# A fused attention and expert kernel: the second dense step in seven-product form, the sums of x shared by VectorE and GpSimd

## The reference

```python
N, D, E, F = (1152, 512, 4, 1024)
p = domain_probs / (domain_probs.sum(-1, keepdims=True) + 1e-09)
out = np.zeros((N, D), dtype=np.float32)
for e in range(E):
    h = np.maximum(x @ w1[e], 0.0)
    out += p[:, e:e + 1] * (h @ w2[e])
```

## Time and profile before

| What | Value |
|---|---|
| Median of 3 runs | 610.3 us (609.96 to 613.1) |
| The profiled execution's own time | 610.63 us |
| Its span in the profile | 608.9 us |
| TensorE busy | 593.7 us, 98% of the span |
| VectorE, ScalarE, GpSimd busy | 346.9, 214.8, 305.4 us |
| Mean granted TensorE clock | 0.999 of full |

### The profile page before, as it was taken

The page is one execution under the profiler, slowest core; times in us unless marked ns, Lnnn a source line. Parts: engine busy times, 40 slices in busy tenths (PEclk is TensorE's granted clock), DMA queues, the critical chain, the costliest instruction groups (busy, mean ns, idle before and its releaser), DMA issues.

```text
span 608.9 us, 10251 instructions
## 1 busy us (share of the span) xinstructions
PE 593.7 (98%) x3607; PEld 524.0 (86%) x3608; DVE 346.9 (57%) x714; ACT 214.8 (35%) x542; POOL 305.4 (50%) x287
## 2 busy tenths in 40 slices
PE   4999999999999999999999999999999999999996
PEld 4898878888888889989889889899899899899894
DVE  4878775248892123785464564554554554654553
ACT  2867732258983231223123123122132132131130
POOL 6546601451110019359996945945756747646005
PEclk9999999999999999999999999999999999999999
DMA  9926556628951002002222112112112011010004
GB/s 213 249 36 238 198 176 236 212 86 302 357 220 35 18 17 71 1 0 70 70 69 71 36 34 70 36 36 69 34 35 69 26 43 60 15 63 0 0 0 155
DMA packets 27252, 56.70 MB, mean 93 GB/s; under 512 B 7000, under 2 KB 9688, under 8 KB 27224
## 3 DMA queue, kind: packets, MB, share of 16 engines
q1 hardware_dynamic: 18792, 31.93, 16.6%
q0 software_dynamic: 6848, 21.52, 10.8%
q10 hardware_dynamic: 1584, 2.88, 1.6%
HBM read 48.97 MB, written 7.36 MB: 93 GB/s over the span
## 4 chain that ended last, share of the span: by engine, by line
PE 91%; POOL 3%; DVE 2%; DMA 2%; issue 1%; ACT 0%; SPq 0%; DVEq 0%; POOLq 0%
PE bank L1618 30%; PE bank L1589 30%; PE bank L1513 10%; PE bank L1499 10%; PE bank L1396 2%; PE bank L1488 2%; POOL out L627 1%; PE bank L1433 1%; PE bank L1359 1%; PE bank L1407 1%; DMA kT<-in_kT 1%; PE bank L1476 1%; PE bank L1482 1%; PE bank L1391 1%; PE bank L1354 1%
## 5 line engine op out<-in xcount | busy, mean ns | idle before, releaser
L1263 DVE SCALAR_TENSOR_TENSOR acc<-bank,meta_s,acc 128x512 f32<-128x512 f32 x135 | 100.8, 748 | 62.2 <-PE bank L1618 62.1
L1618 PE MATMUL bank<-u_hi,h_hi 128*128 128x512 f32 x288 | 112.3, 390 | 0.0
L1618 PE MATMUL bank<-u_lo,h_hi 128*128 128x512 f32 x288 | 112.1, 389 | 0.0
L1618 PE MATMUL bank<-u_hi,h_lo 128*128 128x512 f32 x288 | 112.0, 389 | 0.0
L1310 DVE SCALAR_TENSOR_TENSOR h_lo<-bank,h_hi 128x288 fp32r<-128x288 f32 x112 | 50.9, 454 | 44.7 <-ACT h_hi L811 23.0
L1589 PE MATMUL bank<-x2T_hi,u_hi 128*128 128x288 f32 x232 | 68.4, 295 | 0.0
L1589 PE MATMUL bank<-x2T_lo,u_hi 128*128 128x288 f32 x232 | 68.4, 295 | 0.0
L1589 PE MATMUL bank<-x2T_hi,u_lo 128*128 128x288 f32 x232 | 68.3, 295 | 0.0
L799 ACT COPY part_p<-bank 128x288 f32<-128x288 f32 x28 | 11.2, 400 | 157.9 <-PE bank L1589 157.9
L1589 PE MATMUL bank<-t_hi,u_hi 128*128 128x288 f32 x224 | 66.2, 295 | 0.0
L1589 PE MATMUL bank<-t_lo,u_hi 128*128 128x288 f32 x224 | 66.0, 295 | 0.0
(11 more groups left out here) (235 smaller groups left out, 1222.7 us busy)
## 6 DMA issues: line engine op xcount, KB each, us to landing
w_raw<-in_moe_w SPq DMA_DIRECT2D x20, 1024.0 KB, 7.6
u_raw<-in_moe_w POOLq DMA_DIRECT2D x16, 512.0 KB, 3.8
u_raw<-in_moe_w POOLq DMA_DIRECT2D x16, 256.0 KB, 3.2
u_raw<-in_moe_w POOLq DMA_DIRECT2D x32, 128.0 KB, 2.9
x_tile<-x_by_expert ACTq DMA_DIRECT2D x11, 256.0 KB, 2.7
x_by_expert<-zero_row SPq DMA_DIRECT2D x10, 256.0 KB, 3.1
qT<-in_qT SPq DMA_DIRECT2D x4, 576.0 KB, 9.1
kT<-in_kT SPq DMA_DIRECT2D x8, 288.0 KB, 10.5
```

The source lines that it names most:

```text
L1263: w.scalar_tensor_tensor(out=acc[:, t, :], in0=bank[Z_BANK[i]][:], scalar=meta_s[:, t, bass.ds(e + 1, 1)], in1=acc[:, t, :], op0=ALU.mult, ...
L1618: last = t_.matmul(bank[Z_BANK[i]][:], lhs[:, c, ts], rhs[page][:, c, :], start=c == 0 and k == 0, stop=c == 1 and k == 2)
```

## The change

`PLAIN` becomes 1, so step 1 is a seven-product step too. Its differences of x must be there one step earlier:

- VectorE makes the eight sums of `x_sum[0]` itself, two behind each of four `cut_plain` of step 0, then the four `make_t` of `s = 0`; GpSimd makes only those of `x_sum[1]`, between `split_u1(1)` and `split_u2(1)`.
- VectorE's `split_t(0)` and `make_t(1)` stand between the additions of step 0's nine tiles (`first_z`), and the four `split_t(1)` behind them.
- ScalarE's eight `cut_t` stand behind the last `keep_plain` of step 0.
- `split_u1(1)` now forms the weight sums: four TENSOR_TENSOR, and 1792 in place of 1024 elements in its cast and its subtraction.
- GpSimd no longer waits for `t_split`; TensorE waits for each difference before the product that reads it.

```diff
-    PLAIN = 2
+    PLAIN = 1
...
             pool.wait_ge(g_done, 1)
             split_u1(1)
+            pool.wait_ge(x2_whole, 1)
+            sum_x(1)
             split_u2(1)
-            pool.wait_ge(x2_whole, 1)
-            sum_x(0)
-            sum_x(1)
-            pool.wait_ge(t_split[0], 4)
-            pool.wait_ge(t_split[1], 4)
-
-            for n in range(PLAIN, STEPS2):
-                if n < 2 * PLAIN:
+
+            for n in range(2, STEPS2):
+                if n < 2 + PLAIN:
                     pool.wait_ge(g_done, len(PLAIN_ORDER) * (n - 1))
...
+            def sum_x(k, c):
+                w.tensor_tensor(x_sum[0][:, k, c, :], x2T_hi[:, c, cols_of(0, k)].bitcast(FP32),
+                                x2T_lo[:, c, cols_of(0, k)].bitcast(FP32), ALU.add).then_inc(x_summed[0], 1)
...
+            dve.wait_ge(x2_whole, 1)
             for j in range(1, len(PLAIN_ORDER)):
                 cut_plain(0, j)
...
+                if j <= DC:
+                    sum_x(0, j - 1)
+                    sum_x(1, j - 1)
+                if j == DC:
+                    dve.wait_ge(x_summed[0], 2 * DC)
+                    make_t(0, *order_t[0])
+                elif j > DC:
+                    make_t(0, *order_t[j - DC])
             for i in range(NT):
-                add_z(1, 0, i)
+                first_z(i)
+                if i < 4:
+                    split_t(0, *order_t[i])
+                elif i < 8:
+                    dve.wait_ge(x_summed[1], 2 * DC)
+                    make_t(1, *order_t[i - 4])
+            for at in order_t:
+                split_t(1, *at)
...
+                if first and k >= 4:
+                    pe.wait_ge(t_split[s], T_AT[{5: (0, 0), 7: (1, 0), 6: (1, 1), 4: (0, 1)}[k]])
...
-            pe.wait_ge(t_split[0], 4)
-            pe.wait_ge(t_split[1], 4)
             for n in range(PLAIN, FS):
-                whole_step(n, n - PLAIN, n)
+                whole_step(n, n - PLAIN, n, n == PLAIN)
```

40 lines of the change are left out of this document (15 added, 25 removed).

## The result

The changed kernel takes **631.3 us** in the median of 6 runs (630.55 to 632.96), the kernel before 610.78 (609.96 to 613.1, 6 runs): ratio 1.033, 95% interval 1.0306 to 1.0356. The profiled execution took 631.86 us, with a span of 630.1 us where that of before was 608.9: 21.2 us more.

What follows compares the result with a forecast made beforehand. The prediction took TensorE as the bound, busy all the time at full clock in steps 1 and 2. It summed 610.6 - 1.57 + 0.1 + 12.6 = 621.7, or 621.4 us against the median, range 608.5 to 627.

Steps and rivals of the forecast that it cites:

- split_u1(1), cast and subtraction: VectorE's new sums of x meet GpSimd's cast (1.68) and subtraction (4.06): 5.8 us of waits before free time is taken off.
- GpSimd's eight sums: GpSimd's sums of x against VectorE's alternating two-operand and PSUM operations: about 0.2 left each time, 1.6 us (0 to 6.4).
- split_u2(1): GpSimd's 1.05 and 2.39 us operations behind its sums of x, each under one VectorE PSUM operation of 0.67: 2.1 us.
- weight sums of split_u1(2): GpSimd's four sums for step 2's weights, 0.74 each, delay VectorE by 0.3 us.
- its cast and subtraction: Those of split_u1(2) on GpSimd against VectorE's four split_t(1): 5.1 us (0 if VectorE is through first).
- idle time used up: VectorE's free time before step 0's first tile absorbs 2.3 us of the waits.
- The bound and the removed matmuls: TensorE bounds steps 1 and 2; twelve matmuls fewer in step 1 save 24.97 - 23.40 = 1.57 us.
- The schedule of VectorE left alone: Without interference from GpSimd, VectorE reaches sum_c11 of step 1 at about 253.7.
- the wait of 0 to 0.5: TensorE's wait before step 1's seventh product with each engine left alone: 0.1 us (0 to 0.5).
- only GpSimd waits: Rival: VectorE passes at once, GpSimd is delayed and make_t(1) stalls: 612.5 to 615.5, say 614 us; chance 0.13.
- no contention: Rival: two-operand VectorE instructions and GpSimd's pass each other, not slower: 608.8 to 609.2 us; chance 0.22.
- the change does less: Rival: ScalarE's loop entry or new waits cost TensorE 1 to 2 us, no gain: 610 to 611 us; chance 0.03.

Runs made afterwards that it cites:

- e2: Changed kernel with GpSimd's casts, subtractions and sums of steps 1 and 2 replaced by memsets of about the same length: 609.49 us, ratio 0.999.
- e12b: Separate small kernel varying what precedes GpSimd's row of ten sums; phases 4 and 6 (issue of loads under VectorE's work): longest VectorE sums 8.32 and 7.74 us.
- e13b: Changed kernel with GpSimd issuing step 2's first-layer loads behind its eight sums of x, not ahead of them: 627.15 us, ratio 1.0246.
- e15b: Changed kernel with one added GpSimd semaphore wait, behind the first of its eight sums of x: 628.12 us, ratio 1.0299.
- e3: Changed kernel with a GpSimd semaphore wait for its own last instruction between its sums of x and between its weight sums: 624.53 us, ratio 1.0219.
- e6: Changed kernel with unread extra matmuls, 46 ahead of step 0's fourth tile and 13 ahead of step 1's seventh product: 634.92 us, ratio 1.0404.
- e1: Separate small kernel timing rows of VectorE instructions beside GpSimd rows; two SBUF operands take 1.34 us beside reads, 0.75 beside memsets.
- e8: Changed kernel with step 1's weight sums earlier, GpSimd resting until differences are split, VectorE making all 16 sums of x, ScalarE scaling tiles: 609.4 us, ratio 0.9974.
- e14b: Separate small kernel varying issue, memsets, arrival and gaps around GpSimd's ten sums; longest VectorE sum 8.27 us in phase 5 (one load), 1.64 in 6 (one gap).
- e4: Kernel before the change, with only GpSimd's two waits for t_split ahead of its loop removed: 628.67 us, ratio 1.0302.
- e5: Changed kernel with GpSimd's two waits for the split differences put back ahead of step 2's weights: 621.32 us, ratio 1.0167.

## Why the prediction was wrong in size

The direction, the place and half of the mechanism (two-operand VectorE instructions wait for GpSimd's reads) were right; 631.3 lies above the range, which ended at 627. Term by term, as lateness of VectorE at `sum_c11`; measured is the duration in the timeline of after less the undisturbed one of e2's (0.81 a pair of sums, 0.75 a difference, 2.75 four splits). The idle time is what closes the sum; e2's timeline has gaps of 1.7 us there, and at each of the five some 0.08 of overlap are lost besides:

```
term                                    predicted   measured   from the rows at
split_u1(1), cast and subtraction       5.8         5.0        229.49, 232.09
issue of the loads                      0           0.6        236.68
GpSimd's eight sums                     1.6         5.9        238.41, first of the pair
split_u2(1)                             2.1         2.9        238.41, second; 245.96
weight sums of split_u1(2)              0.3         2.3        249.03, 252.18
its cast and subtraction                5.1         4.3        253.38, 255.83
split_u2(2)                             0           2.4        269.60
idle time used up                       -2.3        -2.3
together (before rounding)              12.6        21.0
```

- **The bound and the removed matmuls** hold: a step is 23.40 us, and e2, without meetings, has a span 1.3 us below that of before.
- **The schedule of VectorE left alone** holds to 0.1 us (e2: 253.79 against 253.7).
- **The step that failed** is "GpSimd's eight sums of 0.80, against VectorE's alternation of one two-operand and one PSUM operation: GpSimd runs under the PSUM operation (0.67), and about 0.2 is left each time: 1.6 (0 to 6.4)". It takes turns for granted, from the step before it, "each can hold the other, for the rest of a whole instruction". The row stood right behind GpSimd's DMA issue, VectorE's sum came 0.13 us behind the row's start, and it waited not for the rest of one instruction but for the row to end: 5.9 us. The upper bound of the term held that, and the prediction names it among what would make it wrong ("GpSimd's short sums win against a waiting VectorE several times in a row"), but it took a value near the other end. e12b shows such a hold in a kernel of its own; e13b and e15b take it away from the eight sums in the changed kernel and get VectorE 4.4 and 4.5 us of it back.
- **This step alone does not carry the time out of the range**: 621.4 and the 4.3 us more are 625.7. The rest came from terms without an upper bound or without any value: the weight sums, `split_u2(2)`, the issue and the clock. The bounds that the terms do state add up to 613 to 627 (1.8 + 0 + 2.1 + 0.3 + 0 and 3.5 + 6.4 + 2.1 + 0.3 + 5.1, with the wait of 0 to 0.5) and not to the "615 to 629" of the prediction, so even with everything at its worst stated value it could not reach 631.3.
- **The weight sums** look like the same thing: the difference at 249.03 starts 0.14 us ahead of three sums that follow an issue of 0.73 us (248.42), and ends at 251.89, behind the gap of 251.26 to 251.34. 2.3 where 0.3 was predicted, with no upper bound given. No run put a gap into this row alone; in e3 it has gaps, and there a difference that comes 0.15 us behind its start takes 1.22 us.
- **`split_u2(2)`** was not in the sum. VectorE was so late that the next step's cast and subtraction (268.43 to 272.79) met the last four splits: 2.4 us. Lateness here brings more lateness.
- **The cast and subtraction of `split_u1(2)`** came near their price by luck. The prediction sets them against the four `split_t(1)`, yet with its own lateness these would have started at about 258.5, behind the end of that subtraction (257.2 by its schedule). They met a difference (253.38) and the first `split_t(0)` (255.83) instead, 4.3 us.
- **The issue**: the pair at 236.68 took 0.6 us more while GpSimd issued three loads. In e2 the same issue stands beside differences that lose nothing, so what this hangs on is open.
- **The clock** was not in it either. TensorE had been idle from 273.1 to 275.90, and the granted clock of the window from 275 is 0.66, half level (1.2 GHz) at first: the twelve matmuls from 275.90 to 278.87 took 2.97 us where the twelve before them went at 0.133 each, 1.6 together. **1.4 us**; among the tiles the low clock cost about 0.5 at most (e6).

The check against the span: the seventh product starts at 275.90, and 254.8 was its time undisturbed: 21.1 us late; with 1.4 of clock, less the 1.57 saved, this gives 20.9, against 21.2 measured.

The rivals: *only GpSimd waits* falls with e1, where both wait; *no contention* with e1 and e2, one with, one without reads; *the change does less* is not what happened, since e2 and e8 show its gain. The Trainium skill, SBUF — State Buffer, section Who interferes with whom, says that a VectorE instruction with two SBUF inputs contends with a GpSimd instruction that reads SBUF and not with one that only writes it. e1 agrees: two SBUF operands take 1.34 us beside reads and 0.75 beside memsets, and with a PSUM operand 0.68, as in e14b where GpSimd runs no sum (12.26).

What stays open: the exact condition of the hold. In all of its cases (238.41 and 249.03 of after, 251.43 of e13b, 252.69 of e15b, phases 4 and 6 of e12b, 5 and 6 of e14b, and the last split of `split_t(0)` in e4) GpSimd's row starts directly behind its own DMA issue, no VectorE sum is being worked on at that moment, and VectorE's instruction starts between 0.51 us ahead of the row and 0.16 us behind it. In phase 0 of e14b a sum was running as the row began (12.86 to 13.31, row at 13.15), in phase 4 it came 0.55 us behind: turns in both. A VectorE sum that waits as a row starts is not held by that alone: in e13b and in phase 5 of e12b, where the row stands behind a subtraction, it is let in. e14b's phases 1 and 2 had turns with a memset between, but whether the memset decided was not tried apart from the arrival. e13b moves the arrival as well as the issue. The profile's spans on GpSimd are rough, so a tenth of a us in these arrivals should not be leaned on.

## What to carry to other kernels

Before moving work, list for each stretch which VectorE instructions have two operands in SBUF and which GpSimd instructions read it, and keep them apart in time: here the two removed waits (e5) were worth 10 us, over six times the 1.57 us of the saved matmuls, and a wait that keeps no one waiting may still hold such pairs apart. Where they must meet, take GpSimd's whole row and not one instruction as the upper bound of VectorE's wait when the row follows a DMA issue, or give the row one semaphore gap; that alone won 3.2 of the 20.5 us here (e15b), keeping the engines apart, with ScalarE's help, won all of them (e8). When a predicted lateness is long, look at what comes next on the holding engine, since late work meets the next step's too.
